# A new hand-written order for the first units and the first dense chunk of an attention and expert kernel

## The reference

```python
# attention: B, H, S, D = 4, 8, 576, 64; factor = 4
out_d = sm_attn(mean4(q), mean4(k), mean4(v))        # softmax attention of the pooled sequence
attn = softmax(where(|i - j| < 4, q @ k.T / 8, -1e9))  # a narrow band around the diagonal
x = repeat4(out_d) + attn @ v                        # then reshaped to 2304 tokens x 512

# dense layers: w_in 512 x 2048, w_out 2048 x 512
h = x @ w_in
g = where(h >= 1, h, where(h <= -1, 0, (h + 1) ** 2 / 4))
y = g @ w_out

# experts: 8 of them, 288 tokens each, assigned by sorted gate logits
logits = y @ w_gate
out[tokens of e] = relu(y[tokens of e] @ w1[e]) @ w2[e]
```

## Time and profile before

| | us |
|---|---|
| three runs | 867.36, 869.98, 869.7 (median 869.7) |
| the profiled execution | 869.2 |
| its span, first to last instruction | 867.4 |
| first product of chunk 0 starts | 57.13 |
| chunk 0 ends, loop of chunks begins | 125.7 |
| PE busy | 820.8 (95%) |
| DVE, ACT, POOL busy | 509.9, 406.8, 333.2 |

### The profile page before, as it was taken

How to read it: one execution, slowest core, us unless ns; L and a number is a source line. 1 busy time by engine, 2 the same in 40 slices (tenths; PEclk the granted TensorE clock), 3 DMA queues, 4 the chain that set the end, 5 groups by cost and what they waited for, 6 DMA issues and landing times. The chain is left out here.

```text
span 867.4 us, 21161 instructions
## 1 busy us (share of the span) xinstructions
PE 820.8 (95%) x7658; PEld 748.8 (86%) x7658; DVE 509.9 (59%) x1424; ACT 406.8 (47%) x1006; POOL 333.2 (38%) x391
## 2 busy tenths in 40 slices
PE   6779999999999999999999999939999999999995
PEld 4668889898889898898999999838999999999995
DVE  4667776655665665563544344366766766766620
ACT  4555655445545553553444444303454454455461
POOL 6570233113302321240000000007687787787882
PEclk9898999999999999999999999957999999999998
DMA  9975421320321333201101000006625625616611
GB/s 198 245 195 153 121 88 45 91 79 22 92 80 44 67 90 80 67 2 39 49 2 49 0 24 2 22 4 222 220 68 185 233 61 202 229 49 219 219 40 45
DMA packets 99301, 85.49 MB, mean 99 GB/s; under 512 B 63664, under 2 KB 71856, under 8 KB 99248
## 3 DMA queue, kind: packets, MB, share of 16 engines
q1 hardware_dynamic: 93808, 74.74, 29.6%
q0 software_dynamic: 3072, 9.44, 3.7%
q10 hardware_dynamic: 2368, 0.59, 0.4%
HBM read 70.60 MB, written 14.16 MB: 98 GB/s over the span
## 5 line engine op out<-in xcount | busy, mean ns | idle before, releaser
L528 PE MATMUL PS<-xs,W 128*128 128x256 f32 x1728 | 234.5, 285 | 1.3 <-DVE xT L432 1.3
L528 PEld LDWEIGHTS PS<-xs,W 128*128 128x128 f32 x1728 | 222.9, 189 | 12.5 <-issue 3.1
L528 PE MATMUL PS<-W,g 128*128 128x512 f32 x864 | 221.3, 394 | 1.5 <-DVE g L660 1.5
L528 PEld LDWEIGHTS PS<-W,g 128*128 128x128 f32 x864 | 153.2, 188 | 30.0 <-DVE g L660 3.2
L633 ACT ACTIVATE scratch<-PS,minus 128x256 f32<-128x256 f32 x144 | 68.4, 475 | 215.3 <-DVE scratch L670 215.3
L670 DVE TENSOR_SCALAR scratch<-PS 128x256 f32<-128x256 f32 x144 | 61.0, 424 | 124.5 <-PE PS L528 123.6
L441 POOL TENSOR_TENSOR P<-P,top 128x640 f32<-128x640 f32 x11 | 13.9, 1262 | 220.8 <-DVE top L391 220.8
L1549 POOL TENSOR_TENSOR w1s<-w1r,w1s 128x512 fp32r<-128x512 f32 x64 | 80.8, 1289 | 28.5 <-ACT w1s L1437 28.2
L1344 PE MATMUL PS<-exs,w1s 128*128 128x288 f32 x256 | 81.2, 317 | 0.0
L1344 PE MATMUL PS<-ehs,w2s 128*128 128x288 f32 x256 | 80.9, 316 | 0.0
L1345 PE MATMUL PS<-exs,w1s 128*128 128x288 f32 x256 | 76.3, 298 | 0.0
(11 more groups left out here) (198 smaller groups left out, 1445.8 us busy)
## 6 DMA issues: line engine op xcount, KB each, us to landing
w1r<-in_moe_w SPq DMA_DIRECT2D x16, 1024.0 KB, 5.0
w2r<-in_moe_w SPq DMA_DIRECT2D x16, 1024.0 KB
vd<-in_v SPq DMA_DIRECT2D x16, 288.0 KB
xt<-xT SPq DMA_DIRECT2D x16, 288.0 KB, 2.2
y<-scratch SPq DMA_DIRECT2D x18, 256.0 KB, 2.1
vw<-in_v SPq DMA_DIRECT2D x34, 128.0 KB, 2.8
scratch<-in_moe_w_in SPq DMA_DIRECT2D x8, 512.0 KB, 5.8
scratch<-in_moe_w_out SPq DMA_DIRECT2D x8, 512.0 KB, 5.1
```

What stands on the lines that cost most here:

```text
L528: r = pe.matmul(psum, wsel(w[i]), xsel(x[j]), start=first and t == 0, stop=last and t == 2)
```

## The change

The loops over early units and the `first=True` branch of the chunk functions are gone. In their place every engine has a straight list of calls, in a new order, up to the end of chunk 0. Helper functions are split so that the halves can stand apart (`dve_centre` into `dve_top` and `dve_centre`, `dve_rden` into `dve_den` and `dve_rden`, `pool_probs` into `pool_p` and `pool_pd`, the chunk bodies into `pe_layer1`, `pe_layer2`, `act_relu`, `act_square`, `act_g`, `dve_clip`). In units 5 and 6 the subtraction of the maximum is `pool_centre` as in the loops, written out. The pieces come in a new order, w_in and w_out in turn, and ten of them are finished on GpSimd. There are 9 identity products in place of 24. The code of the loops after chunk 0 does the same as before.

```diff
-ORDER = [0, 1, 2, 3, 4, 5, 6, 8, 9, 10, 11, 7, 12, 13, 14, 15]
-POOL_PIECES = [1, 3, 5, 6]
-LATER_PIECES = [2, 4, None, None]
-BY_POOL = sorted(POOL_PIECES)
+ORDER = [0, 1, 8, 2, 9, 3, 10, 4, 11, 5, 12, 6, 13, 7, 14, 15]
+BY_POOL = [2, 4, 5, 6, 7, 8, 9, 10, 11, 13]
@@ GpSimd
-                for n in range(EARLY):
-                    pool_vp(pool, n)
-                    if n:
-                        rest_of_first_x(pool, n - 1)
-                    pool_probs(pool, n, small=False)
-                    pool_piece(pool, POOL_PIECES[n])
+                pool_vp(pool, 0)
+                pool_pd(pool, 0, small=False)
+                pool_p(pool, 0, small=False)
+                pool_piece(pool, 2)
...
+                pool_pd(pool, 3, small=False)
+                pool_piece(pool, 5)
+                rest_of_first_x(pool, 3)
+                pool_piece(pool, 6)
+                pool_p(pool, 4)
+                pool_pd(pool, 4)
+                pool_vp(pool, 4)
+                pool_piece(pool, 7)
+                pool_piece(pool, 8)
+                pool_piece(pool, 9)
+                pool_centre(pool, 5)
+                pool_piece(pool, 10)
+                pool_piece(pool, 11)
+                pool_p(pool, 5)
+                pool_vp(pool, 5)
+                pool_pd(pool, 5)
+                pool_piece(pool, 13)
@@ ScalarE (unit 0 and 1; then where chunk 0 begins)
+                act_exp(act, 0)
+                act_piece(act, 1)
+                act_piece(act, 2)
+                act.wait_ge(probsd_turned, 1)
+                act_expd(act, 1, AT[1])
+                act_pT(act, 0, AT[0])
+                act_pdT(act, 0, AT[0])
+                act_exp(act, 1)
+                act_od(act, 0, AT[0])
+                act_piece(act, 3)
...
+                act_relu(act, 0, 0)
+                act_relu(act, 0, 1)
+                act_square(act, 0, 0)
+                act_piece(act, 7)
+                act_pT(act, 4, TM)
+                act_piece(act, 8)
+                act_square(act, 0, 1)
+                act_g(act, 0, 0)
+                act_pdT(act, 4, TM)
+                act_relu(act, 0, 2)
+                act_g(act, 0, 1)
+                act_square(act, 0, 2)
+                act_piece(act, 9)
+                act_od(act, 4, TM)
+                act_g(act, 0, 2)
+                act_relu(act, 0, 3)
+                act_piece(act, 10)
+                act_qT(act, 5, TM)
@@ VectorE (where chunk 0 begins)
+                dve.wait_ge(xs_lo, 3)
+                dve_xT(dve, 3, AT[1])
+                dve_top(dve, 4, TM)
+                dve_centre(dve, 4, TM)
+                dve_den(dve, 4, TM)
+                dve_clip(dve, 0, 0)
+                dve_rden(dve, 4, TM)
+                dve_rdend(dve, 4)
+                dve_clip(dve, 0, 1)
+                dve_g(dve, 0, 0)
+                dve_clip(dve, 0, 2)
+                dve_pT(dve, 4, TM)
+                dve_g_rest(dve, 0, 0)
@@ TensorE (chunk 0)
+                pe_layer1(pe, 0, 0)
+                pe_layer1(pe, 0, 1)
+                wait_piece(pe, 1)
+                pe_layer1(pe, 0, 2)
+                pe_turn_p(pe, 4, TM)
+                pe_layer1(pe, 0, 3)
+                pe_out_local(pe, 4, TM, 2, 0, HALF, NB)
+                pe_turn_pd(pe, 4, TM)
+                pe_out_local(pe, 4, TM, 2, 0, 0, HALF)
+                wait_piece(pe, 2)
+                pe_layer2(pe, 0, 0)
+                pe_out_pooled(pe, 4, TM)
```

More of the change, by code:

```diff
@@ L598, in pe_chunk @@
                     pe_turn_y(pe, c)
-                if s == 1 and not first:
+                if s == 1:
                     if units:
@@ L644, in act_chunk @@
                     act_split_x(act, c + 1)
[L645 to L651 removed]
+                act_units(act, c, units, s)
+            act_y(act, c)
         def dve_g(dve, c, f):
@@ L686, in dve_chunk @@
                     dve_split_x(dve, c + 1)
[L687 to L693 removed]
+                dve_units(dve, c, units, s)
+            dve_y(dve, c)
         xt_rows = xt_dram.rearrange("k p t -> (k p) t")
@@ new lines, in _ @@
+                dve_g_rest(dve, 0, 0)
+                dve_g(dve, 0, 1)
+                dve_clip(dve, 0, 3)
+                dve_xT(dve, 4, TM)
+                dve_g(dve, 0, 2)
+                dve_g_rest(dve, 0, 1)
+                dve_kT(dve, 5, TM)
+                dve_g_rest(dve, 0, 2)
+                dve_clip(dve, 0, 4)
+                dve_pool_q(dve, 5)
+                dve_pool_k(dve, 5)
+                dve_g(dve, 0, 3)
+                dve.wait_ge(mask_ready, 1)
+                dve_mask(dve, 5, TM)
@@ new lines, in _ @@
+                dve_g(dve, 0, 7)
+                dve_g_rest(dve, 0, 6)
+                dve_rdend(dve, 5)
+                dve_clip(dve, 0, 9)
+                dve_pT(dve, 5, TM)
+                dve_g_rest(dve, 0, 7)
+                dve_g(dve, 0, 8)
+                dve_g(dve, 0, 9)
+                dve_clip(dve, 0, 10)
+                dve_clip(dve, 0, 11)
+                dve_g_rest(dve, 0, 8)
+                dve_g(dve, 0, 10)
+                dve_xT(dve, 5, TM)
+                dve_clip(dve, 0, 12)
@@ new lines, in _ @@
+                dve_rden(dve, 6, TM)
+                dve_piece(dve, 14)
+                dve_clip(dve, 0, 15)
+                dve_g_rest(dve, 0, 12)
+                dve_rdend(dve, 6)
+                dve_g(dve, 0, 14)
+                dve_pT(dve, 6, TM)
+                dve_split_x(dve, 1)
+                dve_g_rest(dve, 0, 13)
+                dve_piece(dve, 15)
+                dve_g_rest(dve, 0, 14)
+                dve_g(dve, 0, 15)
+                dve_xT(dve, 6, TM)
+                dve_g_rest(dve, 0, 15)
@@ new lines, in _ @@
+                pe_mask(pe, 1, AT[1])
+                pe_scores(pe, 1, AT[1], onto=True)
+                pe_dscores(pe, 1, AT[1])
+                pe_turn_pd(pe, 0, AT[0])
+                pe_turn_p(pe, 0, AT[0])
+                pe_out_local(pe, 0, AT[0], 0, 0, HALF, NB)
+                pe_out_local(pe, 0, AT[0], 0, 0, 0, HALF)
+                pe_out_pooled(pe, 0, AT[0])
+                pe_turn_pd(pe, 1, AT[1])
+                pe_warm(pe, AT[0] + 3, 3)
+                pe_turn_qk(pe, 2, AT[0], 0)
@@ new lines, in _ @@
+                pe_turn_p(pe, 1, AT[1])
+                pe_mask(pe, 2, AT[0])
+                pe_scores(pe, 2, AT[0], onto=True)
+                pe_out_local(pe, 1, AT[1], 0, 1, HALF, NB)
+                pe_out_local(pe, 1, AT[1], 0, 1, 0, HALF)
+                pe_out_pooled(pe, 1, AT[1])
+                pe_dscores(pe, 2, AT[0])
+                pe_warm(pe, AT[1] + 3, 3)
+                pe_turn_qk(pe, 3, AT[1], 1)
+                pe_mask(pe, 3, AT[1])
+                pe_scores(pe, 3, AT[1], onto=True)
@@ new lines, in _ @@
+                pe_turn_p(pe, 2, AT[0])
+                pe_dscores(pe, 3, AT[1])
+                pe_out_local(pe, 2, AT[0], 1, 0, 0, HALF)
+                pe_turn_pd(pe, 2, AT[0])
+                pe_out_local(pe, 2, AT[0], 1, 0, HALF, NB)
+                pe_out_pooled(pe, 2, AT[0])
+                pe_turn_p(pe, 3, AT[1])
+                pe_warm(pe, TM + 3, 3)
+                pe_turn_qk(pe, 4, TM, 2)
+                pe_out_local(pe, 3, AT[1], 1, 1, 0, HALF)
+                pe_out_local(pe, 3, AT[1], 1, 1, HALF, NB)
@@ new lines, in _ @@
+                pe_layer1(pe, 0, 9)
+                wait_piece(pe, 9)
+                pe_layer1(pe, 0, 10)
+                pe_turn_p(pe, 5, TM)
+                pe_layer2(pe, 0, 5)
+                pe_layer1(pe, 0, 11)
+                pe_turn_pd(pe, 5, TM)
+                pe_out_local(pe, 5, TM, 2, 1, HALF, NB)
+                pe_out_local(pe, 5, TM, 2, 1, 0, HALF)
+                pe_out_pooled(pe, 5, TM)
+                wait_piece(pe, 11)
+                pe_layer1(pe, 0, 12)
+                wait_piece(pe, 8)
```

554 lines of the change are left out of this document (374 added, 180 removed).

## The result

The changed kernel takes 873.9 us (median of 5 runs, 871.8 to 875.4), the kernel before 869.7 (5 runs, 867.4 to 870.0): a ratio of 1.0058, interval 1.0041 to 1.0075. It is slower, where I had forecast 863.8 and the range ended at 869.5. The rival on the slower side had priced 872.3. The profiled execution took 873.25 with a span of 871.5 (869.2 and 867.4 before).

The account below looks back on a forecast made before the run. Early units were taken as bound by byte arrival order, chunk 0 by how soon its first steps start, later by TensorE. -4.2 - 1.1 - 3.3 + 2.2 + 1.0 = -5.4 from 869.2 gave 863.8 us; range 858.5 to 869.5.

Parts of the forecast that it names:

- The rival on the slower side: Chunk 0: GpSimd keeps DVE out through whole runs of pieces, layer 2 at 69 us, total 872.3 us; chance 0.13.
- Pieces on GpSimd, +2.2: Chunk 0 and unit 6: GpSimd finishing seven more pieces holds DVE and ACT at places, net loss of 2.2 us.
- The second place: Pieces 10 and 11 behind `pool_centre`: two DVE holds in a row not hidden, counted as 1.9 us.
- The other two parts of the term: ACT standing at piece 10 for its slot's reload, 1.3 us; one more such place in unit 6, 1.0 us.
- Its second half: Pieces 10 and 11: a DVE hold of 5.7 us less 3.4 of cover, then PE's low clock, another 3 us.
- early gain of 5.3 us: Before the first dense product: 4.2 us from unit 3's earlier transposition and 1.1 from there to the product.
- Transposition of unit 3, -4.2: Early units: with loads and steps reordered, it starts at about 33.5 us instead of 37.65, gaining 4.2 us.
- the rule of arrival: Early loads: each is usable 1.8 us after the running sum of bytes reaches it; `vw` of unit 0 at 21.9 us.
- Fewer identity products, +1.0: Early units: leaving out 15 of 24 costs PE's clock between nothing and 3 us, taken as a 1.0 us loss.
- Unit 3 to the first product, 7.9: Last step before the first dense product: 7.9 us in place of 9.0, gaining 1.1 us.
- Opening of chunk 0: Layer 2 starts 10.1 to 12.3 us into chunk 0 against 15.3; gain of 2.2 to 4.3 us, taken as 3.3.
- The loop of chunks at 119 to 121: After chunk 0: start of the loop of chunks at 119 to 121 us, a sign that the forecast is right.

Follow-up runs that it names:

- e8: Changed kernel with pieces 7 to 11 and 13 finished by DVE instead of GpSimd: 864.4 us, 0.9956 of the kernel before.
- e3: Changed kernel with 16 identity products on PE ahead of layer 2 of block 0: 868.7 us, 1.0008 of the kernel before.
- e4: Changed kernel with GpSimd waiting for `glo` of block 0 before piece 7 and of block 1 before piece 8: 866.9 us, 0.9987 of the kernel before.
- e1: Changed kernel with each GpSimd piece from piece 5 on cut into eight operations of 128 columns: 872.6 us, 1.0059 of the kernel before.
- e2: Changed kernel with 5 identity products before the first transposition and 6 before unit 0's product with v, behind a wait: 869.5 us, 1.0013 of the kernel before.
- e10: e9 with the eleven early identity products of e2 added: 862.8 us, 0.9942 of the kernel before.
- e12: Kernel before with 9 of its 24 early identity products left: 868.7 us, 1.001 of the kernel before.
- e9: e8 with the Relu of block 5 ahead of piece 12 on ACT: 865.0 us, 0.9959 of the kernel before.
- e6: e5 with the Relu of block 5 ahead of piece 12 on ACT: 864.4 us, 0.9955 of the kernel before.
- e7: Changed kernel with `vp` of unit 4 on GpSimd behind pieces 7 and 8 instead of ahead: 869.6 us, 1.001 of the kernel before.
- e5: Changed kernel with the two waits of e4 and the eleven identity products of e2 together: 866.6 us, 0.9976 of the kernel before.

## Why the prediction was wrong

- *The whole.* The forecast was -5.4 us, the measured change +4.1 on the span. The distance of 9.5 splits by the ledger: 2.6 up to the first product (-5.3 forecast, -2.67 measured), 6.4 in chunk 0, where the forecast had -3.3 + 2.2 + 1.0 = -0.1 and the trace shows +6.3 (74.89 for 68.56), and 0.5 behind it. The +1.0 is for identity products that stand in the early units; counted there, the split is 1.6 and 7.4. The split is of one execution of each.
- *Pieces on GpSimd, +2.2: the step that failed.* It said "at most 2.36 a piece if they get in between pieces" and "One held operation is hidden". The conditional was taken for the fact. `glo` of block 0 was held for 5.59 us. The evidence stood in the earlier trace rows and in the text: DVE had not got in between two operations back to back. Against it I had set that ACT delivers the pieces 1.5 us apart; but GpSimd came to them late, from Pd and `vp` of unit 4: it took piece 7 at 63.88, when ACT's share of piece 8 had been done since 62.5. A run without a gap is made by whatever keeps GpSimd away before it. Against the same order with the pieces on DVE (e8) the term measured 9.6 in place of 2.2. The second place, pieces 10 and 11 behind `pool_centre`, was counted as 1.9, and that was about right: there DVE did get in at two boundaries (1.38 and 1.92 us; the third hold, 1.89, ended with piece 11), and PE waited 0.92 and 0.62. The other two parts of the term did not come: ACT copied piece 10 at 75.19 without waiting for its load (1.3 forecast), and a hold of 2.38 beside piece 13, at 100.03, cost PE nothing (1.0 forecast). One reading in the earlier trace rows was of the wrong row: the addition of 0.62 at 87.46 stands beside a step of `vp`; beside the five short operations it is `glo` at 91.19, which took 0.62 as well.
- *The rival.* It had the place (block 0), the time of layer 2 (69; measured 68.90), the clock behind the wait (e3) and the end (872.3; measured 873.9), and got 0.13 of the chance. Its second half failed: at pieces 10 and 11, where it had a hold of 5.7 us, DVE got in between. And its end is near the measured one in part by luck, since it went with an early gain of 5.3 us that came as 2.67. The cause in block 0 is shown: e4 takes the run apart and e8 takes the pieces away, with 0.7 and 1.0% in return, and 7.4 and 9.6 us of chunk 0; e1 shows that it is not the length of an operation. That DVE is kept out through any run is not shown, and the boundaries at which it got in speak against it. That the hold comes from the two engines' reads and writes of SBUF is argued from the earlier trace rows and the page, not shown apart here. The Trainium skill (SBUF — State Buffer, Who interferes with whom) says that whoever has the shared ports keeps them for the whole instruction; the trace goes beyond it: here DVE was kept out for up to seventeen instructions in a row. The 2.91 of the earlier trace rows, which the prediction says agrees with the page, had gone beyond it already, by one instruction.
- *Transposition of unit 3, -4.2: mis-sized, measured -1.35.* `vw` of unit 0 was used at 22.39 (21.9 forecast), so the rule of arrival was right. The products behind it took twice their length until 32 us. From the local product to the transposition it took 13.9 us in the changed kernel, 12.6 to 14.0 in the other eight with the same early code and long rows, and 10.9 in e2 and e10 with short ones. So the long rows account for 1.7 to 3.1 us, about the missing 2.85. What spreads the nine stays open.
- *Fewer identity products, +1.0, "nearer nothing since the early units wait for other engines anyway": mis-sized.* In the old order that holds (e12: no change). In the changed order the chain in the early units is no longer one of waits for bytes but of PE's own rows, and there 11 added products brought the first dense product forward by 2.7 us (e2: 51.78 for 54.46) and 3.3 (e10: 52.28 for e9's 55.60). The two terms are one mistake: the gain of the first was worked out with rows at single length, and the price of losing that length was taken from a kernel with another critical chain. That the 15 products left out are what lost it is not shown.
- *Unit 3 to the first product, 7.9: right* (7.74 from unit 4's transposition to the first product).
- *Opening of chunk 0, layer 2 10.1 to 12.3 us in:* 14.4, the 4.32 of the wait too many; without the hold, 10.1 in e4 and e8.
- *The loop of chunks at 119 to 121* came in e8 (119.75), e9 (120.84) and e6 (119.53).

What stays open: why DVE was let in at some boundaries between GpSimd's operations (pieces 10 and 11, pieces 8 and 9 in e4, piece 8 and `vq` in e7, and all of e1's second run) and at others not. It isn't whether the next piece was ready: ACT's share of piece 11 had been done since 82.1, 2 us before GpSimd began piece 10, and DVE got in ahead of piece 11. Memsets between them are shown not to be enough in block 0, a wait that is stood through is. Whether it depends on which engine's operation was queued first, on operands or on banks wasn't tried. Nor is it settled what keeps PE's rows at double length up to 32 us; that added identity products end it fits e2, e6 and e10 and not e5.

## What to carry to other kernels

Count a GpSimd operation's cost to VectorE not by its own length but by the run it stands in: a VectorE addition or subtraction in SBUF that arrives beside GpSimd operations without a gap may stand to the end of the run, or may be let in at a boundary; both happened here. So ask, of the order, what GpSimd has queued when the urgent addition comes, and break a run by a wait on that addition's result, not by cutting the work smaller. And where a change takes away waits, the filler that was free before may no longer be: price it by the new chain.
